# SiLU in one ScalarE instruction out of PSUM, and gathers ahead of scatters in the expert tiles

## The reference

```
for t in range(768):                          # batch 4, heads 8, head_dim 48
    y[:, :, t] = r_t @ (state + u * k_t v_t)
    state = w * state + k_t v_t
x = y as [3072 tokens, 384]
h = x @ w_in                                  # 384 x 2048
x = (h * (1 / (1 + exp(-h)))) @ w_out         # SiLU, 2048 x 384
logits = x @ w_gate + bias[modality]          # 8 experts
e = argmax(logits); gate = softmax(logits)[e]
out = gate * (relu(x @ w1[e]) @ w2[e])        # 384 x 1024, 1024 x 384
```

## Time and profile before

| | |
|---|---|
| median of 3 runs | 836.06 us (834.84 to 837.5) |
| the profiled execution | 839.43 us |
| its span, first to last instruction | 837.8 us |
| PE busy (matmuls) | 766.8 us, 92% |
| DVE busy | 574.9 us, 69% |
| ACT busy | 403.2 us, 48% |
| POOL busy | 230.7 us, 28% |
| mean granted clock of PE | 0.979 |

### The profile page before, as it was taken

The page is one execution under the profiler, slowest core; times in us unless marked ns, Lnnn a source line. Parts: engine busy times, 40 slices in busy tenths (PEclk is TensorE's granted clock), DMA queues, the critical chain, the costliest instruction groups (busy, mean ns, idle before and its releaser), DMA issues. The chain is left out here.

```text
span 837.8 us, 25279 instructions
## 1 busy us (share of the span) xinstructions
PE 766.8 (92%) x9890; PEld 743.5 (89%) x9890; DVE 574.9 (69%) x1559; ACT 403.2 (48%) x1064; POOL 230.7 (28%) x337
## 2 busy tenths in 40 slices
PE   3599999999999999999999999996969999999983
PEld 2599899989999999999999999996969999999983
DVE  7767886896779677967797777436846655566660
ACT  3355554545454444454444453435445654665650
POOL 4311222152215221522242212102323223333221
PEclk9998999999999999999999999997989999999997
DMA  8911222222222222122222210504556656556650
GB/s 324 409 56 36 71 90 71 91 71 90 72 90 71 89 73 87 53 83 74 83 70 90 72 55 2 189 2 160 138 175 230 239 192 232 216 197 221 226 203 17
DMA packets 24162, 104.93 MB, mean 125 GB/s; under 512 B 4411, under 2 KB 9800, under 8 KB 20482
## 3 DMA queue, kind: packets, MB, share of 16 engines
q1 hardware_dynamic: 19362, 93.30, 31.2%
q0 software_dynamic: 4704, 10.29, 3.8%
HBM read 93.86 MB, written 10.11 MB: 124 GB/s over the span
## 5 line engine op out<-in xcount | busy, mean ns | idle before, releaser
L576 ACT ACTIVATE sig<-ps_h 128x256 f32<-128x256 f32 x192 | 73.2, 382 | 207.3 <-PE ps_h L907 206.5
L905 PE MATMUL ps_h<-x_hi,wi_hi 128*128 128x256 f32 x576 | 167.1, 290 | 0.9 <-DVE g L753 0.9
L906 PE MATMUL ps_h<-x_lo,wi_hi 128*128 128x256 f32 x576 | 163.4, 284 | 0.0
L907 PE MATMUL ps_h<-x_hi,wi_lo 128*128 128x256 f32 x576 | 163.1, 283 | 0.0
L753 DVE TENSOR_TENSOR g<-ps_h,sig 128x256 f32<-128x256 f32 x192 | 81.1, 423 | 92.7 <-ACT sig L576 90.9
L922 PE MATMUL ps_o<-wo_hi,g_hi 128*128 128x392 f32 x384 | 136.3, 355 | 7.6 <-DVE g_lo L757 7.6
L923 PE MATMUL ps_o<-wo_lo,g_hi 128*128 128x392 f32 x384 | 131.4, 342 | 0.0
L924 PE MATMUL ps_o<-wo_hi,g_lo 128*128 128x392 f32 x384 | 131.2, 342 | 0.0
L475 POOL TENSOR_TENSOR store<-store,up_half 128x256 f32<-128x256 f32 x44 | 35.7, 812 | 292.4 <-PE ps_y L892 288.3
L905 PEld LDWEIGHTS ps_h<-x_hi,wi_hi 128*128 128x128 f32 x576 | 110.9, 192 | 4.8 <-DVE g L753 3.1
L907 PEld LDWEIGHTS ps_h<-x_hi,wi_lo 128*128 128x128 f32 x576 | 111.2, 193 | 0.0
(11 more groups left out here) (192 smaller groups left out, 1631.9 us busy)
## 6 DMA issues: line engine op xcount, KB each, us to landing
store<-in_w SPq DMA_DIRECT2D x28, 1536.0 KB, 6.5
store<-in_quads SPq DMA_DIRECT2D x48, 704.0 KB, 4.6
x_rows<-rows SPq DMA_DIRECT2D x12, 384.0 KB, 3.4
wi_raw<-in_wi SPq DMA_DIRECT2D x4, 768.0 KB, 10.6
woT_raw<-in_woT SPq DMA_DIRECT2D x4, 768.0 KB, 12.5
wo_raw<-in_wo SPq DMA_DIRECT2D x4, 768.0 KB, 13.1
store<-x_rows,entries POOLq DMA_INDIRECT x26, 6.2
out_rows<-y,entries_out POOLq DMA_INDIRECT x26
```

Source lines behind the costliest of these rows:

```text
L905: T.matmul(out, hi, x_hi[:, t % 2, c, :], start=(c == 0), stop=False)
L906: T.matmul(out, hi, x_lo[:, t % 2, c, :], start=False, stop=False)
L907: last = T.matmul(out, lo, x_hi[:, t % 2, c, :], start=False, stop=(c == KC - 1))
```

## The change

ACT writes `g` itself, with its SiLU function out of PSUM; the buffer `sig`, its semaphore and DVE's product are gone. `g_high(F)` follows at once in the same slot. On DVE `g_low(F-1)` stands ahead of `add_state` in every slot. `silu(F)` waits until `g_hi` and `g_lo` of slot F - 2 are made, since g has two buffers. As `g_made` no longer comes from DVE, PE gets waits of its own for DVE's reads of the gate's columns and of the ranks.

In the experts, the two gathers leave the function `tile` and stand ahead of `results_out` of the tile before; in the first tile they also stand ahead of the scatters into the lists. The wait for the last rows in `x_rows` goes from SP at the end of the front block to POOL ahead of the first gather.

```diff
-            def sigmoid(F):
+            def silu(F):
                 act.wait_ge(h_made, F + 1)
                 if F >= 2:
-                    act.wait_ge(g_made, F - 1)
-                S.activation(sig[:, F % 2, :], ps_h[F % 2][:, 0:ETOK], ACT.Sigmoid).then_inc(sig_made, 1)
+                    act.wait_ge(g_hi_made, F - 1)
+                    act.wait_ge(g_lo_made, F - 1)
+                S.activation(g[:, F % 2, :], ps_h[F % 2][:, 0:ETOK], ACT.Silu).then_inc(g_made, 1)
...
-                if F > 0 and f == 0:
-                    g_high(F - 1)
                 if F >= 0:
-                    sigmoid(F)
-                if f > 0 and F > 0:
-                    g_high(F - 1)
+                    silu(F)
+                    g_high(F)
...
-            def g_times(F):
-                if F >= 2:
-                    dve.wait_ge(g_lo_made, F - 1)
-                dve.wait_ge(sig_made, F + 1)
-                V.tensor_tensor(g[:, F % 2, :], ps_h[F % 2][:, 0:ETOK], sig[:, F % 2, :], ALU.mult).then_inc(g_made, 1)
-
...
-                    link(V.tensor_tensor(z.picked[:], ps_h[0][:, SIDE:SIDE + RANKS].rearrange("p (n e) -> p n e", e=E),
-                                         z.list_base[:, None].to_broadcast([P, TB, E]), ALU.add))
-                if F > 0 and f == 0:
+                    V.tensor_tensor(z.picked[:], ps_h[0][:, SIDE:SIDE + RANKS].rearrange("p (n e) -> p n e", e=E),
+                                    z.list_base[:, None].to_broadcast([P, TB, E]), ALU.add).then_inc(picks_read, 1)
+                    dve.wait_ge(picks_read, m + 1)
+                if F > 0:
                     g_low(F - 1)
-                if F >= 0:
-                    g_times(F)
                 if F in EVAC_AT and EVAC_AT[F] < LAST_STEP:
                     add_state(EVAC_AT[F])
-                if F > 0 and f > 0:
-                    g_low(F - 1)
...
-                    if F == 1:
-                        pe.wait_ge(gate_lo_made, 1)
+                    if F in GATES_READ_AT:          # {1: 1, 3: 2, 7: 3, 11: 4}
+                        pe.wait_ge(gate_lo_made, GATES_READ_AT[F])
+                    if t >= 2 and t % 2 == 0 and f == RANK + 2:
+                        pe.wait_ge(picks_read, t // 2)
...
-            for i in range(2):
-                sp.wait_ge(rows_out[i], 16 * (TILES // 2))
...
-            def tile(tiles, j, first):
-
+            def gather(j):
                 pool.wait_ge(x_turned, j + 1)
                 pool.sem_inc(pool_passed, 1)
                 for i in range(EB):
                     nc.gpsimd.indirect_dma_start(out=x_in[:, i, :], out_offset=None, in_=z.x_rows,
                                                  in_offset=bass.IndirectOffsetOnAxis(ap=entries[:, i, 0:1], axis=0)).then_inc(x_gathered, 16)
+
+            def tile(tiles, j, first):
...
             pool.wait_ge(entries_in, 16)
+            for i in range(2):
+                pool.wait_ge(z.rows_out[i], 16 * (z.N // ETOK // 2))
+            gather(0)
             tile(z.first_tiles, 0, True)
+            pool.wait_ge(entries_in, 32)
+            gather(1)
             results_out(0)
-
-            pool.wait_ge(entries_in, 32)
             pool.wait_ge(places_made, 1)
...
-            with pool.Fori(1, z.ETILES) as j:
+            tile(table, 1, False)
+            with pool.Fori(2, z.ETILES) as j:
                 with pool.If(j < tiles):
                     pool.wait_ge(entries_in, 16 * (j + 1))
+                    gather(j)
+                    results_out(j - 1)
                     tile(table, j, False)
-                    results_out(j)
+            results_out(tiles - 1)
```

More of the change, by code:

```diff
@@ L234, in front_block @@
     GATES_AT = {-1: 0, 1: 1, 5: 2, 9: 3}
+    GATES_READ_AT = {1: 1, 3: 2, 7: 3, 11: 4}
     FIRST_SLOT, SLOTS = -12, FCH * TILES
@@ L303, in front_block @@
         x_lo = sb("x_lo", [P, 2, KC, ETOK], F32R)
-        sig = sb("sig", [P, 2, ETOK])
         g = sb("g", [P, 2, ETOK])
@@ L362, in front_block @@
         h_made = sem("h_made")
-        sig_made = sem("sig_made")
+        picks_read = sem("picks_read")
         g_made = sem("g_made")
@@ L368, in front_block @@
         rows_made = sem("rows_made")
-        rows_out = [sem(f"rows_out{i}") for i in range(2)]
+        rows_out = z.rows_out
         fill_made = sem("fill_made")
@@ L618, in _ @@
                     S.activation(z.share[:], z.below[:], ACT.Sigmoid).then_inc(share_made, 1)
-            g_high(SLOTS - 1)
             for i in range(EB):
@@ L780, in _ @@
                     if F >= 0:
-                        dve.wait_ge(sig_made, F + 1)
+                        dve.wait_ge(g_made, F + 1)
                     gate_low(GATES_AT[F])
                 if m >= 0 and F == FCH * (2 * m + 2) + RANK:
-                    dve.wait_ge(sig_made, F + 1)
+                    dve.wait_ge(g_made, F + 1)
                     if m == 4:
                         V.tensor_copy(z.n_of[:], ps_h[0][:, SIDE + RANKS:SIDE + RANKS + E])
-                    link(V.tensor_tensor(z.picked[:], ps_h[0][:, SIDE:SIDE + RANKS].rearrange("p (n e) -> p n e", e=E),
-                                         z.list_base[:, None].to_broadcast([P, TB, E]), ALU.add))
-                if F > 0 and f == 0:
+                    V.tensor_tensor(z.picked[:], ps_h[0][:, SIDE:SIDE + RANKS].rearrange("p (n e) -> p n e", e=E),
+                                    z.list_base[:, None].to_broadcast([P, TB, E]), ALU.add).then_inc(picks_read, 1)
+                    dve.wait_ge(picks_read, m + 1)
+                if F > 0:
                     g_low(F - 1)
-                if F >= 0:
-                    g_times(F)
                 if F in EVAC_AT and EVAC_AT[F] < LAST_STEP:
                     add_state(EVAC_AT[F])
-                if F > 0 and f > 0:
-                    g_low(F - 1)
                 if F in SCALE_AT:
@@ L1351, in build @@
         z.first_tiles = sb(whole, "first_tiles", [P, FIRST, 2], I32)
+        z.rows_out = [whole.enter_context(nc.semaphore(f"rows_out{i}")) for i in range(2)]
         with ExitStack() as raw:
```

## The result

The changed kernel takes 809.94 us (median of 4 runs, 808.95 to 810.66) where the kernel before took 836.47 beside it (4 runs, 834.84 to 837.5): 0.9684 of it, 95% interval 0.9664 to 0.9703, or 26.5 us less. The profiled execution took 810.66 us for a span of 809.1.

What follows compares the result with a forecast made beforehand. PE bounds the kernel, so only its waits count: 10.6 + 17.4 - 0.7 + 3.1 + 1.9 = 32.3 us saved, from the 836.06 median to 803.8, predicted 804. Range 795 to 815, with 0.65 for 797 to 810.

Steps and rivals of the forecast that it cites:

- the first rival: Front: table switches fall on PE's path, half of 14 us of loads uncovered, giving 811; chance 0.12.
- front (PE's waits): Attention and dense layer: shorter PE waits at tile ends, before scores and for g save 10.6 us, bounds 4 and 13.4.
- experts, turn's waits, new stall, clock: Experts: all 12 waits for gathered rows go, 17.4 us; 0.7 new stall for w1; 3.1 gained from the clock.
- the one on the clock: Sign of being right: no granted clock of 0.5 from 600 to 820 us.
- that on g_lo: Sign of being right, front: under 4 us of PE idle time before the down steps, which wait for g_lo.
- that on the scores: Sign of being right, front: no wait of PE for scores beyond 1 us.
- ACT has a slot, 2.7 us, before PE needs what it makes ... I take 0.: Front: extra table loads, 14.1 us of ACT time, are mostly covered; cost taken as 0, other end 14.
- The tile ends: Front: g_low(F-1) comes early, g_low(F) is late next; 0.25 of each 0.85 us stall stays, 5.4 us gained.
- The gathers are issued till 729 and land by 735: Steady expert tile: gathers land 8 us before the turn near 743, so all 12 stalls go, 17.4 us.
- the 0.7 put down for w1: First expert tile: w1's split on ACT leaves no slack before PE's matmuls; 0.7 us of new stall.
- The third rival: Experts: weights or entries become the late DMA at the turn, a microsecond in each of 11 tiles, 815; chance 0.07.
- results_out ... behind a loop already left: 0.: End of the kernel: the last results are the same work behind the loop; 0, at best 2 us gained.

Runs made afterwards that it cites:

- e1: Front of the changed kernel with the experts block and the wait for the last rows as in the kernel before; 829.67 us against 836.87, ratio 0.9916.
- e5: Changed kernel with the routing's share also made by Silu, in both blocks, so one table serves; 804.70 us, 0.9631 of the kernel before.
- e9: Changed kernel with g_low(F) of a tile's last slot moved ahead of the scaling on DVE; 812.10 us, 0.9682 of the kernel before.
- e3: Kernel before with only g_low(F-1) moved ahead of the state additions on DVE, sigmoid and product kept; 836.67 us, ratio 0.9989.
- e6: Changed kernel with g_low(F-1) behind the state additions again, except in a tile's first slot; 806.02 us, 0.9652 of the kernel before.
- e10: Changed kernel with a fourth buffer for the entries, loaded one tile earlier; 813.56 us, 0.9712 of the kernel before.
- e7: Changed kernel with the last results_out in a condition nested inside the loop's last full iteration; 814.51 us, 0.9721 of the kernel before.

## Why the prediction was right, and where its steps were off

The forecast was 32.3 us less, 804; it became 26.5, and 809.94 lies within 795 to 815, near the first rival's 811 and only just inside the 797 to 810 that had the chance of 0.65. By parts, forecast and traces:

| part | forecast | measured |
|---|---|---|
| front (PE's waits) | 10.6 | 7.2 (e1); 11.4 by the traces, 3.8 of it chance of the first tile |
| block end | 1.9 | 2.0 |
| experts, turn's waits, new stall, clock | 17.4 - 0.7 + 3.1 = 19.8 | 18.0 |
| end of the kernel | 0, at best 2 gained | 2.6 lost |

Of the signs that it had named for being right, the one on the clock came (it is 1 from 600 to 798 us), that on g_lo (3.0 us) and that on the scores (0.9 at most) too; but two waits for gathered rows were left, and there are 13 table loads, not one or two.

Right in mechanism and size: a Silu at the sigmoid's price (383 ns for 382), the up step's wait for g gone, the block's end, ten of twelve waits of the turn gone, and with the long ones the low clock behind them: at 614.65 six transposes take 0.87 us where they took 1.54, and the matmuls after them stand 0.18 apart, not 0.32.

Four steps failed.

"ACT has a slot, 2.7 us, before PE needs what it makes ... I take 0." The pair of loads was 2.6 us as worked out, and PE did not wait for ACT. But ACT's order has x_high behind it, for which DVE waits at once, and the time comes back at the scores. The forecast had them 3.1 us better and they became about a microsecond worse. e5 gives 5.4 us for it; the rival's price was 7. I had weighed cover by the engine's mean idle time and by PE alone, not by the next instruction in ACT's queue and its reader. This was the largest miss, and it was on the list with a chance of 0.12: the rival was right in the cause, not in the path. It was partly hidden, too. Take the 11.4 us of the traces without the 3.8 of chance, add the 4.5 that e5 gives back, and the front without the loads gains some 12.1 (an estimate), 1.5 more than was forecast. That the sum for the front is only 3.4 off is in part luck.

The tile ends: 5.4 forecast, with 0.25 left of each. They left 0.54 in routing tiles and 0.29 in the others; with the first tile's end, where 0.7 to 1.3 us of idle time stayed, 1.6 to 2.5 us less was gained than forecast. The 0.29 is the 0.25 that was worked out, and the 0.54 is the table loads again: in e5 all these ends have 0.29. That the last g_low behind the scaling would be late next was foreseen, and e9 shows it (5.8 us when it is moved). The moved g_low that was credited with the gain is no part of it (e3, nothing; e6, faster without).

"The gathers are issued till 729 and land by 735": the copy of the entries was put right behind the gather, as if the results' landing took the 2.6 us at most of before. It stands behind that landing, and the results, leaving in the same microsecond as w2 in most tiles, took 4.7 to 7.7 us. The turn moved what the results collide with. It left two waits of 1.3 us; the 0.7 put down for w1 did not come (ACT's split at 609.66 starts without a wait). e10 shows the cause. The third rival had named late entries, with a chance of 0.07 and a microsecond in each of 11 tiles; it came in two tiles here and in five in e7 and e9.

"results_out ... behind a loop already left: 0." The loop is left only after six empty iterations, 2.6 us between y and its results; e7 shows it.

The block's end gave 2.0 for 1.9. Together the parts fall 3.4 + 1.8 + 2.6 - 0.1 = 7.7 us short and the medians 5.8; the 1.9 between is less than the uncertainty of e1 alone (its interval is 2.7 us to either side).

## What to carry to other kernels

When an activation function is changed, look which other functions the engine still calls: each of them may now cost two table loads, and what they cost is read from the next instruction in that engine's queue and who reads it, not from the engine's idle share. A chain of order, wait for landing, copy, load and gather on one queue is a circle: add up one turn of it against the tile, with each landing beside the large transfer that it will then meet. An instruction moved ahead of others is a gain only if its own reader was late; here the ones it passed were the late ones.

## What the runs showed of the hardware

DVE's two-input instructions with both inputs in SBUF took 0.81 to 0.87 us in place of 0.42 while POOL worked off its TENSOR_TENSORs without a gap; those with an input in PSUM kept their time (in the changed kernel x_low takes 1.31 us for three, in 24 places with such work of POOL over most of it and in 11 with none). The Trainium skill, "SBUF — State Buffer", section "Who interferes with whom", says that the first kind contends with POOL's reads of SBUF, one of them blocking until the other is done; the trace agrees on which kind suffers, and its price here is 0.4 us for each instruction. Who began first decides it in the kernel before: in 13 places POOL's product began 0.02 to 0.07 us behind a g_low and the g_low took 0.41 or 0.42 us (the one at 151.42); in seven POOL's was already 0.2 to 0.3 us old and more of its work followed, and the g_low took 0.72 to 0.83 (the one at 182.52).

Two indirect writes of results landed at most 2.6 us after their last issue ahead of a 1.5 MB load of weights (1.75 us in e10), and 4.7 to 7.7 us when they left within 1.2 us of it; in the one tile where they left 4 us behind it they took 1.9.

An empty iteration of POOL's dynamic loop, with one condition, took some 0.43 us (2.6 us for six).

Between 60 and 85 us the granted clock fell to 1.2 GHz for 3.4 us in eight of the 14 profiled executions, twice in seven and once in e3, with PE busy all but 0.05 us of the 25. It did so in one profile of the changed kernel and not in the other, and the first tile's end came 1.8 us later for it. What sets it off was not found.
